# Attention and two expert layers on one core: sums inverted by columns, sink gathers on GpSimd, and other rounds for the first weights

## The reference

```
scores = scale * np.matmul(q, k.transpose(0, 1, 3, 2))      # B, H, S, D = 2, 8, 768, 64
keep = is_sink | in_window                                   # sinks: keys 0 to 3; window: 128
scores = np.where(keep, scores, -1000000000.0)
a = np.exp(scores - np.max(scores, axis=-1, keepdims=True))
a = a / (np.sum(a, axis=-1, keepdims=True) + 1e-09)
x = np.matmul(a, v)                                          # then (B*S, H*D) = (1536, 512)
for e in range(4):
    out += p[:, e:e + 1] * (np.maximum(x @ w1[e], 0.0) @ w2[e])
h = out @ w_in
return (h * np.cos(h)) @ w_out
```

## Time and profile before

| | us |
|---|---|
| median of 3 runs | 867.11 |
| lowest and highest | 866.72, 868.18 |
| the profiled execution | 869.05 |
| its span | 867.3 |
| PE, DVE, ACT, POOL busy over the span | 846.6, 477.3, 458.0, 533.8 |

### The profile page before, as it was taken

One profiled execution on the slowest core, in us unless ns is written; L12 is line 12 of the kernel. 1 busy time (PEld: TensorE's weight loads), 2 busy tenths in 40 slices (PEclk: granted clock), 3 DMA queues, 4 the chain that ended last, 5 costly groups with the idle time before them and its releaser, 6 DMA issues.

```text
span 867.3 us, 13929 instructions
## 1 busy us (share of the span) xinstructions
PE 846.6 (98%) x4756; PEld 753.2 (87%) x4756; DVE 477.3 (55%) x974; ACT 458.0 (53%) x984; POOL 533.8 (62%) x374
## 2 busy tenths in 40 slices
PE   7999899999999999999999999999999999899998
PEld 5777789889889989989989988988898998898997
DVE  4999834334334335733533423438756759756756
ACT  5676743344335236434234334435867869667864
POOL 2677784764755775765565476775484496584460
PEclk9999999999999999999999999999999999999999
DMA  9664222112211211211211311220220220520201
GB/s 211 163 148 118 67 93 97 53 50 94 93 54 49 97 49 49 98 49 49 97 49 49 98 58 49 88 98 1 98 97 1 97 97 2 170 97 2 97 1 73
DMA packets 73155, 67.30 MB, mean 78 GB/s; under 512 B 40608, under 2 KB 46848, under 8 KB 73088
## 3 DMA queue, kind: packets, MB, share of 16 engines
q1 hardware_dynamic: 73088, 66.42, 25.2%
HBM read 62.96 MB, written 3.19 MB: 76 GB/s over the span
## 4 chain that ended last, share of the span: by engine, by line
PE 84%; DVE 9%; issue 4%; ACT 2%; DMA 1%; SPq 1%; DVEq 0%; ACTq 0%
PE scores L1262 10%; PE scores L1266 10%; PE scores L1264 10%; PE scores L1294 9%; PE scores L1292 9%; PE scores L1290 9%; PE bank L1292 5%; PE bank L1294 5%; PE bank L1290 5%; PE bank L1262 3%; PE bank L1264 3%; PE bank L1266 3%; DVE x_lo L926 2%; DVE scores L825 2%; DMA k_nat<-in_k_dram 1%
## 5 line engine op out<-in xcount | busy, mean ns | idle before, releaser
L513 POOL TENSOR_TENSOR w_lo<-w_raw,w_hi 128x512 fp32r<-128x512 f32 x96 | 128.8, 1352 | 186.4 <-ACT w_hi L618 186.4
L1262 PE MATMUL scores<-x_hi,w_hi 128*128 128x384 f32 x528 | 179.3, 340 | 5.9 <-ACT kept L657 2.9
L1266 PE MATMUL scores<-x_hi,w_lo 128*128 128x384 f32 x528 | 178.0, 337 | 0.0
L1264 PE MATMUL scores<-x_lo,w_hi 128*128 128x384 f32 x528 | 177.7, 337 | 0.0
L520 POOL TENSOR_TENSOR w_lo<-w_raw,w_hi 128x1024 fp32r<-128x1024 f32 x48 | 116.8, 2443 | 66.2 <-ACT w_hi L628 66.2
L628 ACT ACTIVATE w_hi<-w_raw 128x1024 fp32r<-128x1024 f32 x48 | 50.6, 1058 | 190.5 <-PE scores L1294 190.5
L1294 PE MATMUL scores<-w_hi,h_lo 128*128 128x512 f32 x384 | 149.7, 390 | 0.0
L1292 PE MATMUL scores<-w_lo,h_hi 128*128 128x512 f32 x384 | 149.7, 390 | 0.0
L1290 PE MATMUL scores<-w_hi,h_hi 128*128 128x512 f32 x384 | 149.4, 389 | 0.0
L1262 PEld LDWEIGHTS scores<-x_hi,w_hi 128*128 128x128 f32 x528 | 100.2, 190 | 8.3 <-issue 7.5
L1034 DVE SCALAR_TENSOR_TENSOR acc<-scores,probs,acc 128x512 f32<-128x512 f32 x56 | 41.8, 749 | 116.3 <-PE scores L1294 116.3
(11 more groups left out here) (125 smaller groups left out, 1593.8 us busy)
## 6 DMA issues: line engine op xcount, KB each, us to landing
w_raw<-in_moe_w_dram SPq DMA_DIRECT2D x32, 1024.0 KB, 5.1
w_raw<-in_moe_w_in_dram SPq DMA_DIRECT2D x8, 1024.0 KB, 5.0
w_raw<-in_moe_w_out_dram SPq DMA_DIRECT2D x8, 1024.0 KB, 5.1
v_nat<-in_v_dram SPq DMA_DIRECT2D x12, 256.0 KB, 3.4
norm<-routing_dram SPq DMA_DIRECT2D x24, 128.0 KB, 3.1
out_dram<-acc SPq DMA_DIRECT2D x12, 256.0 KB, 4.2
k_nat<-in_k_dram SPq DMA_DIRECT2D x11, 256.0 KB, 4.1
q_nat<-in_q_dram SPq DMA_DIRECT2D x11, 256.0 KB, 4.8
```

Source lines behind the costliest of these rows:

```text
L513: nc.gpsimd.tensor_tensor(w1_slots(w1_lo, h % 2, part), w1_part(h % 2, part), w1_slots(w1_hi, h % 2, part).bitcast(F32), ALU.subtract)\
L1262: nc.tensor.matmul(target[:, 0:HALF], w1_hi[:, i, slot, d], x_hi[:, n - 1, d], start=first and d == 0, stop=False, skip_group_check=True)
L1264: nc.tensor.matmul(target[:, 0:HALF], w1_hi[:, i, slot, d], x_lo[:, n - 1, d], start=False, stop=False, skip_group_check=True)
L1266: last = nc.tensor.matmul(target[:, 0:HALF], w1_lo[:, i, slot, d], x_hi[:, n - 1, d], start=False, stop=d == 1, skip_group_check=True)
```

## The change

Nothing is computed differently except that the sums are inverted before they are transposed.

- **Sums.** `invert_sums` now works on `row_sum[:, t]`, 128x8 in SBUF, in even rounds, before `turn_sinks`. A new `copy_inverse` copies the transposed inverses, 8x128, out of PSUM in odd rounds. `store_inverse` and PE's waits use its semaphore `inverse_copied`.
- **Work moved from DVE to POOL.** `gather_sinks`, `sink_keys` and L959 (now `lower_values`), with the same instructions. On POOL `gather_sinks` stands first in its even round, `sink_keys` behind `part_weights` in its odd round, `lower_values` in rounds 3 and 14 (before: 2 and 13 on DVE).
- **Loads.** The keys and queries of tile 3 are loaded ahead of the values of tile 2. `load_first(0)` moves from the start of the loop into its step `t == 2`, behind `place_sinks`, `store_inverse(0)` and the keys and queries of tile 5; `load_second(0)` moves from step 3 to 4.
- **First weights.** POOL's `sum_weights` moves to rounds 5 to 8 and `first_lo` to 10 to 15, ACT's `first_hi` to 9 to 14, `spread_values(1)` from round 7 to 9. `second_hi(0, 0)` and `second_hi(0, 1)` move into round 26, ahead of the last `copy_out`.

```
@@ sync, the loop of the loads
             load_values(1)
+            load_keys(3)
+            load_queries(3)
+            load_values(2)
             sp.dma_start(probs_in[:], domain_probs.rearrange("(t p) e -> p t e", p=P)).then_inc(probs_landed, 16)
-            load_values(2)
-            for t in range(T + 2):
-                if t == 0:
-                    load_first(0)
+            for t in range(1, T + 2):
                 if 3 <= t < T:
                     load_values(t)
...
                 if t % TPB == 1 and t < T:
                     place_sinks(t // TPB)
-                if t == 3:
+                if t == 2:
+                    load_first(0)
+                if t == 4:
                     load_second(0)
@@ gpsimd
-            spread_values(0)
             for i in range(ROUNDS + 3):
+                if i % 2 == 0 and 0 <= (i - 2) // 2 < T and later((i - 2) // 2):
+                    gather_sinks((i - 2) // 2)
                 if 0 <= i - TURN_LAG < ND:
                     part_weights(i - TURN_LAG)
-                if i == 7:
+                if i == 0:
+                    sink_keys(0)
+                    sink_keys(1)
+                    spread_values(0)
+                elif i % 2 == 1 and (i + 3) // 2 < T:
+                    sink_keys((i + 3) // 2)
+                if i in (3, 2 * TPB + 2):
+                    lower_values(i // TPB // 2)
+                if i == 9:
                     spread_values(1)
-                if 3 <= i < 7:
-                    sum_weights(0, i - 3)
-                if 8 <= i < 14:
-                    first_lo(*divmod(i - 8, 3))
+                if 5 <= i < 9:
+                    sum_weights(0, i - 5)
+                if 10 <= i < 16:
+                    first_lo(*divmod(i - 10, 3))
@@ scalar
-                if 7 <= i < 13:
-                    first_hi(*divmod(i - 7, 3))
+                if 9 <= i < 15:
+                    first_hi(*divmod(i - 9, 3))
...
+                if i == ND + 2:
+                    second_hi(0, 0)
+                    second_hi(0, 1)
             copy_out(T - 1)
 
-            second_hi(0, 0)
@@ vector
             def invert_sums(t):
 
+                dve.wait_ge(exp_ready, H * (t + 1))
+                nc.vector.tensor_scalar(row_sum[:, t], row_sum[:, t], 1e-9, None, ALU.add).then_inc(sums_ready, 1)
+                dve.wait_ge(sums_ready, t + 1)
+                nc.vector.reciprocal(row_sum[:, t], row_sum[:, t]).then_inc(inverse_ready, 1)
+
+            def copy_inverse(t):
+
                 dve.wait_ge(sink_turned, t + 1)
                 if t >= 2:
                     dve.wait_ge(inverse_stored[t % 2], 16 * (t // 2))
-                nc.vector.tensor_scalar(inverse[:, t % 2], sums_bank[0:H, P:2 * P], 1e-9, None, ALU.add)\
-                    .then_inc(sums_ready, 1)
-                dve.wait_ge(sums_ready, t + 1)
-                nc.vector.reciprocal(inverse[:, t % 2], inverse[:, t % 2]).then_inc(inverse_ready, 1)
...
+                nc.vector.tensor_copy(inverse[:, t % 2], sums_bank[0:H, P:2 * P]).then_inc(inverse_copied, 1)
@@ tensor, turn_sinks
                 if t >= 1:
-                    pe.wait_ge(inverse_ready, t)
+                    pe.wait_ge(inverse_copied, t)
                 else:
                     pe.wait_ge(first_ready, 4)
-                pe.wait_ge(exp_ready, H * (t + 1))
+                pe.wait_ge(inverse_ready, t + 1)
```

85 lines of the change are left out of this document (42 added, 43 removed).

## The result

| | before | after |
|---|---|---|
| median, us (8 runs each) | 867.2 | 861.25 |
| lowest and highest | 865.86, 869.88 | 859.12, 865.52 |
| span of the profiled execution | 867.3 | 858.3 |
| that execution's own time | 869.05 | 860.06 |

The ratio is 0.9935, with a 95% interval of 0.9912 to 0.9958. The kernel became faster, as forecast, but by 6.0 us in the median where 13.0 were forecast, and the time lies just above the range (861.0).

A forecast was written before the change was run, and what follows sets the result against it. The attention stage was taken as bound by PE, with DVE's stalls on top. 5.0 + 4.5 - 0.7 + 0.6 + 2.0 + 1.6 = 13.0 us off the 867.3 span gave 854.3, median 854.1; range 851.0 to 861.0.

The forecast's parts named there:

- The loads' 5.0: Ahead of round 5: PE's 3.34 us wait for tile 3's keys and 1.7 of half clock go, 5.0 together.
- DVE's relief of 4.5: Rounds 5 to 23: of 5.5 us of PE stalls from a late DVE, 4.5 come back, bounds 2.5 and 5.5.
- the 61.4: Rounds 5 to 23: the time PE alone needs, 65.0 us at its pace less 3.6 for rounds lacking work.
- The 1 us that ACT was to keep for itself: Rounds 5 to 23: ACT comes near PE's round and keeps about 1 of the 5.5 us of stalls.
- POOL late on the first weights, 0.7: Round 7: PE stalls for tile 2's gather behind POOL's weight wait, between nothing and 2.5 us, taken as 0.7.
- POOL is late: Rival, chance 0.17: weights land at 29 or later or gathers cost more, PE waits for sink weights; 857.6 us.
- Rounds 23 to 24, 0.6: Round 23 to 24: DVE reaches the maskings earlier, shortening PE's wait for exponentials by 0.6 us, bounds 0 and 1.2.
- POOL's added work: Attention rounds: gathers cost POOL 0.5 us a tile, sink keys 0.2; POOL full in rounds 10 to 15, barely late.
- the 1.4: POOL's gathers and sink keys: us for a tile if the skill's factor of two held; POOL's ordinary pair then 6.0.
- The end, 2.0 and 1.6: End of the rounds: moved roundings cut PE's pause by 2.0 us, and no clock fall gives 1.6; bounds 2.0 and 3.7.
- From the span to the median, 3.1: Whole kernel: the span's gain of 13.0 us was taken off the median of 867.11 as well, giving 854.1.
- Slower: Rival, chance 0.04: POOL's gathers ahead of its selections in every even round set the pace; 875 us.

The follow-up runs named there:

- sum later: The changed kernel with sum_weights, first_lo, first_hi and spread_values(1) one round later: 0.9864, 856.76 us.
- later tokens: later second with the first roundings of the tokens one round later on ACT and DVE: 0.9837, 855.36 us.
- the loads alone: The kernel before with only the new order of loads and the new rounds of the first weights: ratio 0.9965.
- early second: first early with the second megabyte of weights put behind the norm weights on SP: 0.9847, 855.84 us.
- later second: sum later with the second megabyte of weights put behind the norm weights on SP: 0.9857, 857.65 us.
- gathers back: The changed kernel with only gather_sinks back on DVE: 0.9899, 860.17 us.
- sinks back: The changed kernel with gather_sinks, sink_keys and lower_values all back on DVE: 0.9868, 856.64 us.
- first early: The changed kernel with the first weights loaded one step earlier on SP, ahead of place_sinks: 0.9866, 857.67 us.
- end alone: The kernel before with only the two roundings of the second weights moved into round 26: ratio 0.998.
- roundings back: The changed kernel with the two roundings of the second weights back behind the last copy_out: 0.9937, 863.09 us.
- sums alone: The kernel before with only the sums inverted by columns on DVE, then transposed: ratio 0.9975.
- early tokens: early second with the first roundings of the tokens one round later on ACT and DVE: 0.9845, 856.09 us.

## Why the prediction was wrong, step by step

The steps of the forecast against the profiled span:

| step | forecast | measured |
|---|---|---|
| start of round 5 | 20.5 | 20.46 |
| rounds 5 to 23 | 66.93 - 4.5 + 0.7 = 63.1 | 66.60 |
| round 23 to 24 | 2.85 | 3.24 |
| round 24 to PE's restart | 12.1 | 12.20 |
| from there to the end | 755.8 | 755.8 |
| span | 854.3 | 858.3 |

The 755.8 of the last step agrees only because the clock fell near 735 us in the profiled executions of both kernels; in *sum later* and *later tokens*, where it didn't, that stretch takes 754.3 and 754.2.

**The loads' 5.0: right**, 5.0 measured. The bounds hid that it needs DVE's relief too: the loads alone gave 2.55.

**DVE's relief of 4.5: right in size.** Round 7 took 7.62 us here and 3.36 in *sum later*, so the stall and the half clock cost 4.3. 66.60 less 4.3 is 62.3, that is 66.93 less 4.6. This is a subtraction and no measurement: in kernels without the stall the eighteen rounds took from 61.3 (*early second*) to 64.1 us (*later second*), by how late POOL was in them. The 61.3, with a wait of 0.68 in it, bears out the 61.4 at which the forecast put PE alone. The 1 us that ACT was to keep for itself is there in number only: the wait of 1.04 before round 23 came from ACT's wait of 1.65 for POOL's `t_sum`, and it is absent in *gathers back* and *sinks back*, where that wait is absent. DVE was busy for 46.38 of the 60 us from 30 to 90, 77% where "near 75%" was forecast.

**POOL late on the first weights, 0.7: this is the step that failed.** Its chain was right link by link: issue between 21 and 22 (21.65), landing between 26 and 29 (29.2, a little beyond), a wait of 3 to 6 (5.41), a gather done between 28 and 31 (30.98), PE asking near 28.5 (28.65), a stall between nothing and 2.5 (2.47). Two things were wrong in what was made of it. The 0.7 is about what the middle of each link gives (landing at 27.5, one sum and the gather, 29.3, less 28.5; the text doesn't say so). The load landed 1.7 later than that middle, and since nothing had slack in this chain, all of it went to PE. And the stall was priced without the clock. The same prediction had read in the earlier trace rows that both pauses of more than 2 us were followed by half clock at 1.7 each, and it did not put that to its own upper end, which should have been 4.2, not 2.5. The stall cost 4.3 instead of 0.7; that alone is 3.6 of the 4.0, and rounds 23 to 24 are the other 0.4. So the mechanism was in the forecast, and the term was sized at its mild end.

The rival "POOL is late" was the true case, in its first condition, a landing at 29 or later; in the full rounds PE waited for sink weights only once, 0.49 us in round 13. Its 857.6 stands for a span of 857.8, against 858.3. What should have raised its chance stood in the text: a strict order, with an instruction in it that waits for a transfer issued late, and behind it one that PE asks for in the same round or so.

**Rounds 23 to 24, 0.6: too much.** 0.2 measured, 3.24 us. Where ACT didn't wait for `t_sum` of the full POOL this step took 2.76 (*sinks back*), 2.77 (*gathers back*) and 2.67 (*later tokens*), which would have been the 0.6 and a little more. PE's wait for exponentials before round 24 is not that wait: it is 0.89 here and still 0.77 to 0.87 in those three.

**POOL's added work: right by the row, wrong by the count.** The gathers took 0.24 and 0.25 us when nothing disturbed them, 0.5 for a tile as forecast and not the 1.4 that the forecast worked out beside it. The Trainium skill (GPSIMD Engine Reference, section 4.1, Engine selection) puts GpSimd at about twice VectorE's time with two inputs. The 1.4 took this twice of 0.48, a row that held DVE's waits for POOL: with POOL idle DVE does the same subtraction in 0.19 (last section). Against that, 0.25 is 1.3 times, so at this small shape the traces don't bear the factor of two out. The same selections and product as before took 0.64 and 1.27 where the forecast had 0.73 and 1.52, so POOL's pairs were also a little lighter than counted.

But the count of POOL's work stopped at round 15. Rounds 17 to 20 have `sum_tokens`, four instructions of 1.8 us, which the kernel before also had and the forecast left out:

```profile
69.67 1.83 POOL L579 TENSOR_TENSOR t_sum<-x_t 128x768 f32<-128x768 f32 x1
71.44 0.24 POOL L491 CAST sink_w<-weights 128x64 fp32r<-128x64 f32 x1
...
73.22 1.28 POOL L529 TENSOR_TENSOR x_t<-x_t,norm 128x512 f32<-128x512 f32 x1
74.46 1.81 POOL L582 TENSOR_TENSOR x_t<-x_t 128x768 f32<-128x768 f32 x1
...
77.55 1.82 POOL L585 TENSOR_TENSOR t_sum<-x_t 128x768 f32<-128x768 f32 x1
79.31 0.24 POOL L491 CAST sink_w<-weights 128x64 fp32r<-128x64 f32 x1
```

The pair of rounds 18 and 19 has two of them and takes POOL 7.9 us from gather to gather (71.44 to 79.31), without a gap, against PE's 7.1; the pairs on either side have one each and take 6.0 and 5.9. So the sums don't make POOL late, but they leave it little room to catch up before ACT asks for the last of them: it waits 1.65 us for it, until 84.12. From 30 to 90 POOL was busy for 56.8 of 60 us, where it was for 45.1 before, and so a wait that it has anywhere ahead of there (5.41 for the weights, 3.28 for the norm weights in *first early*) can come out at PE or, by `t_sum`, at ACT.

**The end, 2.0 and 1.6: right**, 1.88 and 1.57 (from PE's restart to the end 757.4 before and 755.8 after), and *end alone* and *roundings back* show both. The 1.6 is not certain in the kernel before, though: in *sums alone* the same pause of 2.38 us left the clock at 1.00.

**From the span to the median, 3.1.** The forecast took the offset of one profiled execution of before, 1.9 above its median, over to the new kernel. Measured, the profiled run of after lies 1.2 below its own. The spans of its eight runs reach from 857.4 to 863.8, those of the highest with a granted clock of 0.994, of the lowest 0.998. With falls of the clock that come in some runs and not in others, a single profiled execution says little about its place among the rest, and the forecast needed bounds of about 2 us on either side of this offset. It had none.

**Slower**, POOL setting the pace of every pair: nowhere. Most even rounds take 3.73 us, most odd ones 3.37, and the slowest behind round 7 take 4.4 (22) and 4.0 (13).

## What to carry to other kernels

An instruction that waits for a transfer carries everything behind it on its engine. Before moving work to another engine, ask which waits already stand in that engine's order ahead of the moved work, and how late what they wait for may land; the same work was worth 0.6% here when the wait was absent and cost 2.1 us or more (a quarter of a per cent, 0.67% by the ratios) when it was there. A stall of about 2 us or more on TensorE is to be priced with the half clock that may follow, whether it is one that goes or one that comes. And terms that were measured one by one don't add up when they meet in one queue: the parts alone gave 12.2 us, give or take 4, together 5.6.

## What the runs showed of the hardware

**A short DVE instruction can be held for a whole run of POOL instructions.** The clearest case is in *early tokens*. DVE, and below it POOL in the same stretch:

```profile
53.75 4.29 DVE L926 TENSOR_SCALAR row_sum<-row_sum 128x8 f32<-128x8 f32 x1
58.07 0.20 DVE L928 RECIPROCAL row_sum<-row_sum 128x8 f32<-128x8 f32 x1
```

```profile
53.74 1.27 POOL L520 TENSOR_TENSOR v_low<-v_diagonal,v_sink 32x512 fp32r<-32x512 f32 x1
54.98 1.80 POOL L555 TENSOR_TENSOR w_lo<-w_sum,w_hi 128x768 fp32r<-128x768 f32 x1
56.76 1.25 POOL L529 TENSOR_TENSOR x_t<-x_t,norm 128x512 f32<-128x512 f32 x1
```

The addition on 128x8 takes 0.16 us undisturbed (at 19.88 in the changed kernel). Here it began 0.01 us behind a POOL instruction and ended at 58.04, 0.03 after the third of three that followed one another without a gap; PE waited 1.90 for it. In the changed kernel the same line took between 0.16 and 1.36, and its mean of 472 ns, above the forecast, is this. The other long ones told of above (2.47, 1.69, 1.42) are gathers on DVE, from SBUF to SBUF as well. The reciprocal of the same shape, right behind, took 0.20 us each time.

All traces together say the same. Fourteen kernels have this addition, twelve times each. In 29 of the 168 cases POOL ran nothing beside it, and it took 0.16 to 0.17 us; in the other 139 it took 0.16 to 4.29, 0.55 on the mean. The subtraction of the gather on DVE took 0.19 in all 5 cases with POOL idle and 0.58 on the mean of 59 others. *Gathers back* shows it while POOL waits for the weights, DVE and then POOL:

```profile
27.35 0.19 DVE L907 CAST sink_w<-weights 128x64 fp32r<-128x64 f32 x1
27.57 0.19 DVE L910 TENSOR_TENSOR sink_w<-weights,sink_w 128x32 fp32r<-128x32 f32 x1
```

```profile
29.32 1.28 POOL L527 TENSOR_TENSOR w_sum<-w_raw 128x512 f32<-128x512 f32 x1 [4.66 <-DMA w_raw<-in_moe_w_dram]
```

So the 0.47 and 0.48 of the earlier trace rows, which the forecast took for the price of this work on DVE, were for the greater part waits for POOL. The Trainium skill (SBUF — State Buffer, section Who interferes with whom) says that of a VectorE and a GpSimd instruction that both need the shared port, the first has it for its whole instruction and the other fully blocks. The rows agree on the blocking and show that it can last over three instructions in a row; that the port is the reason no run here shows by itself. So a full POOL doesn't only delay its own work, it also makes DVE's short instructions long. By how much goes only roughly with POOL's load: the mean of the addition was 342 ns in *sums alone*, 282 in *sinks back*, 472 in the changed kernel and 525 in *gathers back*, with POOL busy for 47.5, 52.6, 56.8 and 55.9 of the 60 us from 30 to 90.

**The half clock after a pause is not certain.** Near 735 us all kernels have a pause of PE of about 2.6 us before `keep_2`: 2.65 in the changed kernel, until 733.60, and 2.63 in *sum later*, until 730.93. The stretch around the end of the pause in the one, then in the other:

```profile
733.00:738.00 5.00, 4.40 (x17) 4.43 (x18) 2.43 (x5) 3.46 (x8) 4.70 (x4) 0.68 0.58 184
```

```profile
730.00:735.00 5.00, 4.07 (x23) 4.10 (x24) 2.86 (x6) 4.42 (x10) 4.67 (x3) 1.00 0.63 194
```

Mean clock 0.68 and 1.00 behind pauses that differ by 0.02 us and follow and precede the same work. Over the sixteen experiments and the two kernels it fell in ten profiled executions and didn't in eight. Elsewhere in the same executions it fell behind all five pauses of 2.98 to 4.85 us for the keys of tile 3, behind those of 2.47 and 3.38 in round 7 but not behind 2.40, and behind four of the five of 2.38 at the end of the rounds. It fell once behind 1.90 (*early tokens*, 0.73 from 60 to 65 us) and not behind 1.83 (*first early*). After the pauses of 0.49 us it never fell. What decides in between isn't settled here; for an estimate from these cases, a pause of 2.6 us costs its length plus 1.6 to 1.7 us about every second time. That alone gives runs of one kernel a scatter of some microseconds, and no profile of one run shows its mean.
